# Preparing only the first half of w_in during the attention, in half-size pieces

## The reference

```
# 1 attention: batch 2, 8 heads, 768 tokens, head size 64; 4 sink keys and a window of 128
scores = where(is_sink | in_window, scale * q @ k.T, -1e9)
a = exp(scores - max) ; a = a / (sum(a) + 1e-9) ; x = (a @ v) as (1536, 512)
# 2 dense layer: w_in (512, 2048), w_out (2048, 512)
h = x @ w_in ; g = h - tanh(h) ; x = g @ w_out
# 3 mixture of 8 experts, the best 2 of each token by noisy logits: w1 (8, 512, 1024), w2 (8, 1024, 512)
logits = x @ w_gate + log1p(exp(x @ w_noise)) * noise
out[tokens of e] += weight * (relu(x @ w1[e]) @ w2[e])
```

## Time and profile before

| | |
|---|---|
| median of 3 runs | 709.51 us (708.34 to 709.69) |
| profiled execution, time | 710.72 us |
| profiled execution, span | 709.0 us |
| mean granted TensorE clock | 0.995 |
| attention | to about 83 us, then `hidden(0, 0)` |
| PE busy | 98% of the span |
| POOL, ACT, DVE busy from 30 to 80 us | 47.16, 46.27, 42.28 of 50 us |

### The profile page before, as it was taken

One profiled execution on the slowest core, in us unless ns is written; L12 is line 12 of the kernel. 1 busy time (PEld: TensorE's weight loads), 2 busy tenths in 40 slices (PEclk: granted clock), 3 DMA queues, 4 the chain that ended last, 5 costly groups with the idle time before them and its releaser, 6 DMA issues.

```text
span 709.0 us, 12253 instructions
## 1 busy us (share of the span) xinstructions
PE 697.2 (98%) x3530; PEld 566.9 (80%) x3531; DVE 361.3 (51%) x821; ACT 218.7 (31%) x503; POOL 442.3 (62%) x272
## 2 busy tenths in 40 slices
PE   7999999999999999999999999999999999999997
PEld 5666788888888888888887888888888888888885
DVE  4788642222344222442266756556665565555654
ACT  7799632221422223322251212111211221122111
POOL 8899999000004000048569979969994999975472
PEclk9899999999999999999999999999999999999999
DMA  8743368000003000035183588687787987856677
GB/s 278 295 150 101 113 222 327 0 1 1 1 0 119 0 1 0 0 120 191 59 306 110 196 292 263 227 279 249 259 267 222 305 264 263 274 184 203 212 245 254
DMA packets 70257, 121.49 MB, mean 171 GB/s; under 512 B 8272, under 2 KB 36048, under 8 KB 69712
## 3 DMA queue, kind: packets, MB, share of 16 engines
q1 hardware_dynamic: 28272, 63.66, 26.8%
q10 hardware_dynamic: 38112, 44.84, 18.5%
q0 software_dynamic: 3840, 12.59, 5.5%
HBM read 81.74 MB, written 39.32 MB: 171 GB/s over the span
## 4 chain that ended last, share of the span: by engine, by line
PE 88%; POOL 4%; DVE 4%; another core or an unknown queue 1%; issue 1%; ACT 1%; DMA 0%; SPq 0%; DVEq 0%; POOLq 0%
PE bank L1784 23%; PE bank L1739 22%; PE bank L1597 18%; PE bank L1648 18%; POOL arena L735 2%; POOL arena L745 2%; DVE arena L1114 1%; PE bank L1543 1%; DVE arena L1136 1%; PE bank L1552 1%; PE bank L1751 1%; PE bank L1518 1%; PE bank L1670 1%; POOL arena L738 0%
## 5 line engine op out<-in xcount | busy, mean ns | idle before, releaser
L716 POOL TENSOR_TENSOR ring<-ring_raw,ring 128x2048 fp32r<-128x2048 f32 x32 | 147.7, 4615 | 2.5
L770 POOL DMA_INDIRECT sorted_x<-y_rows,arena x24 | 23.5, 978 | 184.2 <-DVE arena L1248 177.8
L1784 PE MATMUL bank<-ring,hidT_hi 128*128 (+1 forms) x448 | 138.3, 390 | 0.0
L714 POOL TENSOR_TENSOR ring<-ring_raw,ones 128x2048 fp32r<-128x2048 f32 x32 | 115.3, 3604 | 30.8 <-DMA ring_raw<-in_moe_w 30.7
L1739 PE MATMUL bank<-ring,xsT_hi 128*128 x464 | 124.3, 390 | 0.0
L1648 PE MATMUL bank<-gated_hi,w_out_sb 128*128 128x512 f32 x384 | 118.6, 390 | 0.0
L1739 PEld LDWEIGHTS bank<-ring,xsT_hi 128*128 128x128 f32 x464 | 87.0, 188 | 18.2 <-issue 0.3
L1182 DVE TENSOR_TENSOR bank<-bank,arena 128x512 f32<-128x512 f32 x48 | 33.6, 699 | 129.1 <-ACT arena L915 127.9
L1784 PEld LDWEIGHTS bank<-ring,hidT_hi 128*128 128x128 f32 x448 | 83.9, 188 | 17.3
L1784 PE MATMUL bank<-ring,hidT_lo 128*128 (+1 forms) x224 | 87.2, 389 | 0.0
L1648 PEld LDWEIGHTS bank<-gated_hi,w_out_sb 128*128 128x128 f32 x384 | 71.9, 188 | 14.8
(11 more groups left out here) (222 smaller groups left out, 1008.5 us busy)
## 6 DMA issues: line engine op xcount, KB each, us to landing
ring_raw<-in_moe_w SPq DMA_DIRECT2D x48, 512.0 KB, 5.3
hid_by_lane<-hid ACTq DMA_DIRECT2D x28, 512.0 KB
hid_lanes<-hid_by_lane ACTq DMA_DIRECT2D x28, 512.0 KB
ring_raw<-in_moe_w SPq DMA_DIRECT2D x8, 1024.0 KB, 6.9
sorted_y<-ys ACTq DMA_DIRECT2D x30, 256.0 KB
xs<-sorted_x ACTq DMA_DIRECT2D x100, 64.0 KB
sorted_y<-zeros SPq DMA_DIRECT2D x1, 4864.0 KB, 24.7
w_in_raw<-in_moe_w_in SPq DMA_DIRECT2D x2, 2048.0 KB, 10.3
```

The costliest lines, as they stand in the source:

```text
L714: pool.tensor_tensor(hi, raw, one_like(raw), ALU.mult).then_inc(rounded, 1)
L716: ins = pool.tensor_tensor(lo, raw, hi.bitcast(F32), ALU.subtract)
L770: pool.indirect_dma_start(out=sorted_x[:, :], out_offset=bass.IndirectOffsetOnAxis(ap=row_at[k][:, kk:kk + 1], axis=0), in_=y_rows_all[:, ...
L1784: last = pe.matmul(bank[into][:, :], x[:, c * P:(c + 1) * P], ring[:, bass.ds(at * 2 * WE + (w + CH * FE + c * DM), DM)], start=c == 0 and ...
```

## The change

Pieces of w_in become half as large, 512 columns, so the 8 pieces that are rounded and split in the attention are its first half. The 8 pieces of the second half are done in block 0 of the dense layer: on ScalarE two roundings behind each of `block_round(0, 2)` to `block_round(0, 5)`, on GpSimd one split behind each of the w_out splits 2 to 9. TensorE waits for 8 pieces before step 0 and for 16 before step 8. Transfers, their order, and VectorE's work are the same.

```diff
-        WIDE = WE // PAIRS
+        WIDE = WE // (2 * PAIRS)
...
                 for fc in range(lo, hi):
                     splits += 1
                     split(w_out_raw[:, fc, 1, :], w_out_sb[:, fc, 0, :], w_out_sb[:, fc, 1, :], splits, w_out_split)
+                    if 2 <= fc < 2 + PAIRS:
+                        split_w_in(PAIRS + fc - 2)
...
                 block_round(0, fc)
                 if fc < 2:
                     attn_out(PAIRS - 1, fc)
+                elif fc < 2 + PAIRS // 2:
+
+                    round_w_in(PAIRS + 2 * (fc - 2))
+                    round_w_in(PAIRS + 2 * (fc - 2) + 1)
...
                 if isinstance(blk, int) and fc % HALF == 0:
 
-                    pe.wait_ge(w_in_split, CH * (fc // HALF + 1))
+                    pe.wait_ge(w_in_split, PAIRS * (fc // HALF + 1))
```

## The result

| | before | after |
|---|---|---|
| median of 5 runs | 708.34 us (707.74 to 709.69) | 714.03 us (712.85 to 715.52) |
| ratio after / before, 95% interval | | 1.007 [1.0051, 1.0089] |
| profiled execution: time, span | 710.72, 709.0 us | 712.85, 711.1 us |
| start of `hidden(0, 0)` | 82.84 | 84.28 |

The kernel became slower by 5.7 us in the medians, 5.0 were forecast. Lines up to 758 keep their numbers, so GpSimd's L724, L735 and L745 are the same; the L1597 of before is L1603, L1543 is L1549, L859 is L861, L1114 is L1120.

A forecast was written before the change was run, and what follows sets the result against it. It took TensorE as the bound, with a chain of waits through GpSimd, TensorE and VectorE in the attention. Terms 0 + 3.43 + 1.6 + 0 gave +5.0 us on a median of 709.51: 714.5 us, range 712.1 to 716.9.

The forecast's parts named there:

- Half-size pieces in the attention: Attention: GpSimd's split shrinks from 2.36 to 1.29 us, but neither it nor the rounding is in the chain: 0.
- The gate: Start of hidden(0, 0): TensorE waits for the eighth split, queued behind the last pair's normalisation on GpSimd: +3.43 us.
- The clock: After TensorE's idle time before step 0, its clock falls and the following matmuls run slower: +1.6 us, bounds 0 and 2.9.
- Rival A: Behind the wait before step 0 the clock stays up, leaving +3.4 us alone, 712.9 us; chance 0.23.
- The second half of w_in: Dense layer, block 0: the moved roundings and splits stay hidden, finishing 0.6 us before hidden(0, 8) needs them: 0.
- Rival B: hidden(0, 8) finds the sixteenth split unfinished: +0.8 us, 715.3, or up to 717.3; chance 0.09 on top of the clock falling.
- Rival C: GpSimd's split held the attention's turns back, so they shorten by up to 7.5 us in all: 707.0 us; chance 0.03.

The follow-up runs named there:

- run 1: The kernel before, with step 0 of the up-projection waiting for all 8 whole pieces of w_in instead of 4: 715.36 us against 708.74, ratio 1.0084.
- run 2: The changed kernel with its eighth w_in piece rounded and split one place earlier, ahead of the last normalisation: 708.84 us against 708.74 for the kernel before, ratio 0.9998.
- run 4: The changed kernel with ScalarE's roundings of w_in's second half one step later: 721.1 us against 708.74 for the kernel before, ratio 1.0167.
- run 6: The changed kernel with one extra GpSimd product of 128x512 zeros in each of pairs 2 to 8: 713.84 us against 708.55 for the kernel before, ratio 1.008.
- run 3: The changed kernel with 15 unused 128x512 matmuls on TensorE ahead of step 0: 711.99 us against 708.74 for the kernel before, ratio 1.0041.
- run 5: The kernel before with one extra GpSimd product of 128x512 zeros in each of pairs 2 to 8: 711.07 us against 708.55, ratio 1.0028.
- run 10: The changed kernel with the eighth w_in piece rounded and split earlier and two VectorE attn_out steps moved: 709.66 us against 709.48 for the kernel before, ratio 1.0001.

## Why the prediction was right

- **Half-size pieces in the attention: 0.** Right. Turns of 9.50 against 9.52, the freed time went into idle time of the two engines. The split's price of 1.29 us was 1.28.
- **The gate: +3.43.** Right: 3.44 us idle, released by GpSimd's L724; on the common scale of the account +3.5. Run 1 makes it alone, run 2 removes it and with it the whole loss.
- **The clock: +1.6.** Right in size, partly by luck: I had taken a little over the middle of 0 to 2.9. In the length of step 0 it cost 1.6 us in the changed kernel (4.59 against 2.95), 1.5 in run 1 (4.44), 2.5 in run 4 (5.46; 2.8 up to step 2), 1.7 at run 4's second gate (4.41 against 2.72), and nothing in run 6. In run 3, with the wait filled, the clock was at 1.00. Since it was so in run 6 with the wait unfilled, that one trace proves little; the medians, 3.3 us above before with the wait filled and 5.7 without, speak for the clock as well. Rival A, that the clock stays up, turned out to be the other of two outcomes: it held in one of the four executions profiled with an unfilled first gate. The trace agrees with the penalty rule of the Trainium skill (TensorE: Matmul & The Clock Gate, "HAM oscillation — how this bites in real kernels") for these dense matmuls: the slices sum to about 3.4 us at the low level, half of which is 1.7, against 1.64 measured. It fits less well in run 4, where half of 6.8 us is 3.4, against 2.8 lost up to step 2. It does not agree that such a pause always has this price (run 6).
- **The second half of w_in: 0.** Right, narrowly as said: room of 0.7 us, GpSimd's new wait of 10.5 us (10.4 forecast). Rival B did not happen; run 4 shows that the gate binds as soon as that room is gone: 5.44 us more of delay gave a wait of 4.8.
- **Rival C, a shorter attention.** Out. Its argument, that GpSimd is 94% busy, is what run 5 tests: it had 0.64 us of slack a turn. Nor was VectorE slowed by GpSimd's work: its masks on 128x260 take 422 ns on average before and 421 in the changed kernel.

The forecast for the median, 714.5, came out 0.5 above the measured 714.03. That it is so close is in part luck: it added 5.0 us to a median of 709.51, while the kernel before came to 708.34 over five runs, and the change cost 5.7; errors of 1.2 and 0.7 us partly cancel. Of those 0.7, the two traces account for 0.1 (3.5 + 1.6); where the rest lies, in the start-up's scatter or in low stretches like run 4's, stays open. What the forecast did not see is the scatter of the start-up, about 2 us between executions; had I compared the two profiled spans alone, the change would have seemed to cost 2.1 us.

## What to carry to other kernels

An engine that is 94% busy need not be the bound: look at whether it stands idle right behind the work in question, and for whom. When work is cut into smaller pieces and a counter's threshold moves with them, ask where the last piece that the threshold now needs stands in its queue; here it stood behind the last link of the stage before, and moving that one piece one place earlier removed the whole loss. A wait of TensorE of a few us costs its length and, mostly but not always, 1.5 to 2.8 us more for the clock in these runs.

## What was unexpected of the hardware

The same order of work does not always bring the same clock. In eight of the twelve profiled executions TensorE pauses 1.5 us near 15 us; in that pause or up to 0.9 us behind it the clock fell in three of them (at 15.4 us before, 16.8 in run 5, 17.3 in run 10) and stayed at 1.00 there in the other five, the changed kernel among them. In runs 1, 3 and 4 it fell earlier, at 12.3 to 13.4 us, behind a pause of only 0.7 to 0.8 us. A pause of 3.4 us before step 0 was followed by a fall in the changed kernel and in run 4, and not in run 6, though the same work stood around it; behind those of 4.5 and 4.8 us (runs 1 and 4) it fell both times. The prediction's clock term thus has no fixed value: in these traces it was 0 to 2.8 us for the same gate.
